# Routing's parts between the experts' products set further apart, VectorE's lower parts of the inner rows behind routing's answers, and GpSimd's fetches moved to match

## The chip, the cores and the metric

The kernel runs on one core of one Trainium2 chip. The metric is the device time of one execution in microseconds (us), the median of the runs shown. TensorE, VectorE, ScalarE and GpSimd each work through a queue of their own in order and wait for each other at semaphores; a wait holds everything behind it on its engine.

## The reference

Attention with a local window and eight global keys, then a dense layer pair with SiLU, then a layer of 8 experts to which 3072 tokens are assigned greedily. The last part, cut to what matters:

```python
logits = x @ w_gate                      # 3072 tokens, 8 experts, cap = 3072 / 8 = 384
order = np.argsort(-logits.flatten())
for idx in order:                        # best pairs first
    tok, e = idx // E, idx % E
    if assigned[tok] >= 0 or counts[e] >= cap:
        continue
    assigned[tok] = e
    counts[e] += 1
for e in range(E):                       # D = 512, F = 1024
    mask = assigned == e
    out[mask] = np.maximum(x[mask] @ w1[e], 0.0) @ w2[e]
```

## The kernel before

The first block (attention and the dense layers) ends at about 709 us and is not touched. The second block, `routed_experts`, computes the experts in the order in which they fill up, so that an expert can be computed while the next are still being routed.

**Products.** An expert is 56 products on TensorE, numbered m = 0 to 55 (`MM`). The first 32 are up products: inner row f = 0 to 7 (128 of the 1024 inner values) by four pieces of D. The last 24 are down products: token tile t = 0 to 2 by f = 0 to 7. A product is three matmuls, since float32 values are split in a high part (rounded) and a lower part (what is left): high by high, high by low, low by high. Product n of the whole run is p * 56 + m for expert p.

**Inner rows.** When inner row f is complete (product 4f+3), ScalarE writes `hidden_high` (L1585) and VectorE `hidden_low` (L1815, in `rest_hidden`). They share three PSUM banks (`UP_BANKS`), so inner row f+3 waits for `hidden_low` of f, and down product 32+f reads it.

**Routing.** Round r finds the next expert that fills, in 22 parts k: seven levels, each a count (even k, TensorE L1416; answered on VectorE by `find_reached`) and a digit (odd k, TensorE L1425; answered by `move_key` and `compare`, which writes `cmp` for the next count), then wins (`WINS`, answered by `fill`, which gives the weights' index), the sum of marks (`SUMS`, `list_them`), three parts on VectorE alone (`MARK` and two halves of `one_hot`), the list (`LIST`, 24 matmuls L1450, answered by `keep_list`, which gives the tokens' index), and `NEXT` and `KEY`, which prepare the next round on VectorE. Levels 0 to 3 have wide compares (31 values), 4 to 6 narrow ones (15 or 17). Round 0 is done before expert 0; rounds 1 to 7 stand between the products of experts 0 to 5, by a table of gaps: `gaps_of(r)` gives for each part how many products after the part before it stands. `parts_behind` maps a product's number to its parts. TensorE does them behind that product in `between`, and VectorE's queue has their answers in the same places, in `decide`.

**Tokens.** From expert 2 on the tokens of an expert are turned (transposed, L1484) in two halves between the down products of the one before, behind m = 39 and 47 (47 and 51 in expert 1); expert 1's are turned at its own start. ScalarE rounds them (L1566), VectorE writes `ex_low` (L1810, in `rest_tokens`), and product 0 waits for that.

**Fetches.** GpSimd writes the lower parts of the weights (`w_low`, L1358 for w1 and L1373 for w2) and issues the indirect DMAs for the next expert between them: w1 (L1334), the tokens (L1350, three issues) and w2 (L1340). `fetch_early(p, f)` sets in front of which of w2's eight rows f the first two stand; each waits for routing's index.

## Time and profile before

| | |
|---|---|
| median of 3 runs | 1079.76 us (1079.34 to 1079.78) |
| profiled execution, its time | 1080.13 us |
| its span, first to last instruction | 1078.4 us |
| granted TensorE clock, mean over the span | 0.987 |
| the experts' products | 751.0 us to the end |

The span lies inside the profiled execution's own time, 1.7 us shorter. PE is TensorE's matmuls and PEld its weight loads, DVE is VectorE, ACT ScalarE, POOL GpSimd. In a timeline row the bracket behind an instruction gives the idle time of the engine before it and what released it. Matmuls overlap, so the distance from start to start is the pace, not the duration.

### The profile page before, as it was taken

The page shows a single profiled execution, that of the slowest core. Times are in us where ns is not written, and L with a number is a line of the kernel's source. Part 1 is how long each engine was busy: PE and PEld are TensorE (multiplying, and loading weights), DVE is VectorE, ACT ScalarE, POOL GpSimd, SP SyncE. Part 2 cuts the span into 40 slices and gives each one's busy share as a digit, 9 for nine tenths or more (in the row PEclk, how much of TensorE's full clock was granted, in tenths as well). Part 3 has the DMA queues.
Part 4 walks back from the last instruction along what each step waited for, and adds up shares of the span by engine and source line. Part 5 has one row for each costly group of instructions (what it writes and reads, how often), then busy time and mean ns, then how long its engine had stood idle before and what let it go on. Part 6 is the DMA issues. An engine that isn't in the chain of part 4 may idle for free. (4 is left out here: it accounts for less than half of the span.)

```text
span 1078.4 us, 19852 instructions
## 1 busy us (share of the span) xinstructions
PE 1035.2 (96%) x7291; PEld 888.8 (82%) x7291; DVE 615.9 (57%) x2248; ACT 460.4 (43%) x1172; POOL 422.3 (39%) x466
## 2 busy tenths in 40 slices
PE   9899999999999999999999999957899999999998
PEld 7688888888888888888888889846677877779987
DVE  6754736474646556564747462546767768774110
ACT  4775444444444444444444443212233334234442
POOL 1363222222222222222222224214476577667773
PEclk9999999999999999999999999977999999999999
DMA  6653212121112120112112000005055245324420
GB/s 185 224 209 119 75 53 70 56 75 45 62 55 75 53 70 30 59 56 76 56 62 69 11 31 2 19 21 186 1 215 182 95 153 184 140 98 171 161 108 29
DMA packets 23248, 98.15 MB, mean 91 GB/s; under 512 B 3008, under 2 KB 5056, under 8 KB 20960
## 3 DMA queue, kind: packets, MB, share of 16 engines
q0 software_dynamic: 9824, 58.99, 15.3%
q1 hardware_dynamic: 13328, 37.90, 10.5%
q8 instruction: 58, 0.95, 0.4%
q14 instruction: 38, 0.31, 0.1%
HBM read 84.30 MB, written 12.85 MB: 90 GB/s over the span
## 5 line engine op out<-in xcount | busy, mean ns | idle before, releaser
L427 POOL TENSOR_TENSOR g_low<-g,g_high 128x256 fp32r<-128x256 f32 x192 | 155.3, 809 | 471.4 <-ACT g_high L646 471.3
L536 PE MATMUL up_ps<-x_high,w_high 128*128 128x256 f32 x768 | 227.6, 296 | 0.0
L536 PE MATMUL up_ps<-x_low,w_high 128*128 128x256 f32 x768 | 216.2, 281 | 0.0
L536 PE MATMUL up_ps<-x_high,w_low 128*128 128x256 f32 x768 | 215.1, 280 | 0.0
L814 DVE SCALAR_TENSOR_TENSOR g<-g,up_ps 128x256 f32<-128x256 f32 x192 | 80.4, 419 | 235.6 <-ACT g L639 235.6
L646 ACT ACTIVATE g_high<-g 128x256 fp32r<-128x256 f32 x192 | 80.3, 418 | 209.4 <-PE down_ps L549 140.3
L536 PEld LDWEIGHTS up_ps<-x_high,w_high 128*128 128x128 f32 x768 | 144.5, 188 | 10.7 <-issue 7.7
L549 PE MATMUL down_ps<-w_high,g_high 128*128 128x512 f32 x384 | 152.1, 396 | 0.0
L549 PE MATMUL down_ps<-w_high,g_low 128*128 128x512 f32 x384 | 151.4, 394 | 0.0
L549 PE MATMUL down_ps<-w_low,g_high 128*128 128x512 f32 x384 | 151.2, 394 | 0.0
L536 PEld LDWEIGHTS up_ps<-x_low,w_high 128*128 128x128 f32 x768 | 144.7, 188 | 2.8
L536 PEld LDWEIGHTS up_ps<-x_high,w_low 128*128 128x128 f32 x768 | 144.9, 189 | 0.0
L802 DVE CUSTOM_DVE_ANT_0 product<-x,w_raw 128x512 bf16<-128x512 f32 x176 | 132.8, 754 | 3.0
L639 ACT ACTIVATE g<-up_ps 128x256 f32<-128x256 f32 x192 | 73.4, 382 | 101.2 <-PE up_ps L536 99.3
L1373 POOL TENSOR_TENSOR w_low<-w_raw,w_high 128x512 fp32r<-128x512 f32 x64 | 82.1, 1288 | 58.3 <-ACT w_high L1561 58.1
L604 ACT ACTIVATE probs<-probs,neg_max 128x232 f32<-128x232 f32 (+1 forms) x184 | 85.1, 463 | 43.7 <-DVE neg_max L734 43.7
L1504 PE MATMUL eup_ps<-ex_high,w_high 128*128 128x384 f32 x256 | 91.3, 357 | 1.4 <-DVE ex_low L1810 1.4
L549 PEld LDWEIGHTS down_ps<-w_high,g_low 128*128 128x128 f32 x384 | 71.9, 187 | 17.7
L1504 PE MATMUL eup_ps<-ex_high,w_low 128*128 128x384 f32 x256 | 86.0, 336 | 0.0
L1504 PE MATMUL eup_ps<-ex_low,w_high 128*128 128x384 f32 x256 | 86.0, 336 | 0.0
L1358 POOL TENSOR_TENSOR w_low<-w_raw,w_high 128x512 fp32r<-128x512 f32 x64 | 80.1, 1287 | 3.6 <-ACT w_high L1554 3.4
L1521 PE MATMUL edown_ps<-w_high,hidden_high 128*128 128x512 f32 x192 | 79.5, 414 | 0.0
(217 smaller groups left out, 1826.5 us busy)
## 6 DMA issues: line engine op xcount, KB each, us to landing
qk_t<-qk_rows SPq DMA_DIRECT2D x20, 720.0 KB, 4.2
v_w<-v_win SPq DMA_DIRECT2D x40, 232.0 KB
w_raw<-weights SPq DMA_DIRECT2D x16, 512.0 KB, 5.4
x_rest<-x_any POOLq DMA_DIRECT2D x24, 256.0 KB, 3.0
x_rows<-x POOLq DMA_DIRECT2D x12, 512.0 KB, 3.2
w_raw<-gate_rows SPq DMA_DIRECT2D x1, 2048.0 KB, 6.8
qk_t<-qk_rows SPq DMA_DIRECT2D x3, 512.0 KB, 4.2
v_w<-v_win SPq DMA_DIRECT2D x8, 128.0 KB
```

The source lines that it names most:

```text
L427: pool.tensor_tensor(g_low[:, u % 2, :], g[:, u % 2, :], g_high[:, u % 2, :].bitcast(F32), ALU.subtract)\
L536: last = nc.tensor.matmul(up_ps[:, u % 2, 0:GT * P], a[:, f, w], x[:, grp % 2, c, :], start=k == 0, stop=k == 3 * C - 1)
L549: last = nc.tensor.matmul(down_ps[:, t, :], a[:, m % 2, t * P:(t + 1) * P], x[:, f, C * P:], start=f == 0 and k == 0, stop=f == FC - 1 and ...
L604: nc.scalar.activation(probs_of(u)[:, a, 0:width], probs_of(u)[:, a, 0:width], ACT.Exp, bias=neg_max[:, u % 3, a:a + 1], scale=-1.0, accum ...
L639: nc.scalar.activation(g[:, u % 2, :], up_ps[:, u % 2, 0:GT * P], ACT.Tanh, scale=0.5)\
L646: nc.scalar.activation(g_high[:, u % 2, :], g[:, u % 2, :], ACT.Copy).then_inc(g_high_ready, 1)
L802: v.tensor_tensor_reduce(out=product[:, :], in0=x2[:, t, :], in1=gate_all[:, e, :], scale=1.0, scalar=0.0, op0=ALU.mult, op1=ALU.add, accu ...
L814: v.scalar_tensor_tensor(g[:, u % 2, :], g[:, u % 2, :], 1.0, up_ps[:, u % 2, 0:GT * P], ALU.add, ALU.mult).then_inc(g_ready, 1)
L1358: pool.tensor_tensor(w1_low[:, f, :], w1_raw[:, p % 2, f, :], w1_high[:, f, :].bitcast(F32), ALU.subtract).then_inc(w1_low_ready, 1)
L1373: pool.tensor_tensor(w2_low[:, f, :], w2_raw[:, f, :], w2_high[:, f, :].bitcast(F32), ALU.subtract).then_inc(w2_low_ready, 1)
L1504: last = nc.tensor.matmul(up_ps[:, f % UP_BANKS, 0:CAP], w[:, f, c * P:(c + 1) * P], x[:, c, :], start=k == 0, stop=k == 3 * C - 1)
L1521: last = nc.tensor.matmul(down_ps[:, t, :], h[:, f, at], w[:, f, :], start=f == 0 and k == 0, stop=f == FC - 1 and k == 2)
```

## The change

The table of gaps is set anew: round 1's last levels have gaps of 2 where they had 1; from round 2 on the first count stands 5 products behind `KEY` instead of 4, from round 4 on 6; from round 4 on also the sixth count stands one product later and the list 3 products behind the last mark instead of 2. All parts behind a changed gap move with it: round 2's by 4 products, round 3's by 5, round 4's by 7 to 9, round 5's by 11 to 13, round 6's by 15 to 17, round 7's by 17 and 18. VectorE's `rest_hidden` now comes behind the answers at its product and one product later (4f+4 instead of 4f+3). GpSimd's early fetches stand in front of later rows of w2.

```diff
--- before.py
+++ after.py
@@ -1286,10 +1286,11 @@
 
 
         def gaps_of(r):
-            ends = [2, 3] + [3, 1, 1] + [2, 1, 2]
+            ends = [2, 3] + [3, 1, 1] + [3 if r >= 4 else 2, 1, 2]
             if r == 1:
-                return [2, 2] + [3, 1] * (UPPER - 2) + [2, 1, 3, 1] + [2, 1] * (NL - UPPER - 1) + ends
-            return [4, 2] + [3, 2] * (UPPER - 2) + [2, 2, 3, 2] + [2, 2] * (NL - UPPER - 1) + ends
+                return [2, 2] + [3, 1] * (UPPER - 2) + [2, 2, 3, 2] + [2, 2] * (NL - UPPER - 1) + ends
+            late = int(r >= 4)
+            return ([5 + late, 2] + [3, 2] * (UPPER - 2) + [2, 2, 3 + late, 2] + [2, 2] * (NL - UPPER - 1) + ends)
 
         parts_behind = {}
         behind = -1
@@ -1361,9 +1362,9 @@
             def fetch_early(p, f):
 
 
-                if p + 1 < E and f == {0: FC, 1: 5, 2: 4, 3: 2}.get(p, 1):
+                if p + 1 < E and f == {0: FC, 1: 6, 2: 5, 3: 4}.get(p, 3):
                     fetch_w1(p + 1)
-                if p + 1 < E and f == {0: FC, 1: FC, 2: 6, 3: 5}.get(p, 3):
+                if p + 1 < E and f == {0: FC, 1: FC, 2: 7, 3: 6, 6: 3}.get(p, 5):
                     fetch_tokens(p + 1)
 
             def rest_w2(p):
@@ -1825,10 +1826,11 @@
                     rest_tokens(p, 0)
                     rest_tokens(p, 1)
                 for m in range(MM):
-                    if m < FC * C and m % C == C - 1:
-                        rest_hidden(p, m // C)
                     for r, k in parts_behind.get(p * MM + m, ()):
                         decide(r, k)
+
+                    if 0 < m <= FC * C and m % C == 0:
+                        rest_hidden(p, m // C - 1)
                     if turned_behind(p, m) is not None:
                         rest_tokens(p + 1, turned_behind(p, m))
```

On VectorE, in the first products of expert 0: `short` and `enough` answer a count of round 1, `digit`, `notes_ps` and `cmp` a digit, `hidden_low` is the lower part of an inner row. Before:

```order
1387 L1664 TENSOR_TENSOR short<-places,route_ps 31x8
1388 L1664 TENSOR_TENSOR short<-short,route_ps 31x8 x2
1389 L1671 TENSOR_TENSOR enough<-route_ps,short 31x8
1390 L1815 SCALAR_TENSOR_TENSOR hidden_low<-eup_ps,hidden_high 128x384
1391 L1676 TENSOR_REDUCE digit<-route_ps 128x1
1392 L1684 TENSOR_SCALAR notes_ps<-notes_ps,digit 128x24
1393 L1650 TENSOR_TENSOR cmp<-notes_ps,qk_t 128x16x31
1394 L1650 TENSOR_TENSOR cmp<-notes_ps,qk_t 128x8x31
1395 L1664 TENSOR_TENSOR short<-places,route_ps 31x8
1396 L1664 TENSOR_TENSOR short<-short,route_ps 31x8 x2
1397 L1671 TENSOR_TENSOR enough<-route_ps,short 31x8
```

And in the changed kernel:

```order
1387 L1665 TENSOR_TENSOR short<-places,route_ps 31x8
1388 L1665 TENSOR_TENSOR short<-short,route_ps 31x8 x2
1389 L1672 TENSOR_TENSOR enough<-route_ps,short 31x8
1390 L1677 TENSOR_REDUCE digit<-route_ps 128x1
1391 L1685 TENSOR_SCALAR notes_ps<-notes_ps,digit 128x24
1392 L1651 TENSOR_TENSOR cmp<-notes_ps,qk_t 128x16x31
1393 L1651 TENSOR_TENSOR cmp<-notes_ps,qk_t 128x8x31
1394 L1816 SCALAR_TENSOR_TENSOR hidden_low<-eup_ps,hidden_high 128x384
1395 L1665 TENSOR_TENSOR short<-places,route_ps 31x8
1396 L1665 TENSOR_TENSOR short<-short,route_ps 31x8 x2
1397 L1672 TENSOR_TENSOR enough<-route_ps,short 31x8
```

The lower part of inner row 0 stood ahead of the answer to the digit; now it stands behind that answer and its two compares, ahead of the answer to the next count.

On TensorE, at the end of expert 0 and the start of expert 1: `route_ps` rows are routing's parts, the 9 and 3 matmuls with `ident` turn expert 1's tokens. Before:

```order
3897 L1416 MATMUL route_ps<-wants,cmp 128x32 x6
3898 L1521 MATMUL edown_ps<-w_high,hidden_high 128x512
3899 L1521 MATMUL edown_ps<-w_low,hidden_high 128x512
3900 L1521 MATMUL edown_ps<-w_high,hidden_low 128x512
3901 L1484 MATMUL eup_ps<-ident,x_g 128x128 x9
3902 L1484 MATMUL edown_ps<-ident,x_g 128x128 x3
3903 L1504 MATMUL eup_ps<-ex_high,w_high 128x384
3904 L1504 MATMUL eup_ps<-ex_low,w_high 128x384
```

And in the changed kernel:

```order
3896 L1522 MATMUL edown_ps<-w_high,hidden_high 128x512
3897 L1522 MATMUL edown_ps<-w_low,hidden_high 128x512
3898 L1522 MATMUL edown_ps<-w_high,hidden_low 128x512
3899 L1426 MATMUL route_ps<-enough,qk_t 128x8
3900 L1485 MATMUL eup_ps<-ident,x_g 128x128 x9
3901 L1485 MATMUL edown_ps<-ident,x_g 128x128 x3
3902 L1505 MATMUL eup_ps<-ex_high,w_high 128x384
3903 L1505 MATMUL eup_ps<-ex_low,w_high 128x384
```

A count of round 2 stood ahead of expert 0's last product; now a digit of that round stands behind it, directly ahead of the turn, and the count that it leads to comes three products into expert 1 (VectorE answers in the same order).

On GpSimd, in expert 2: `w_low` with L1373 (now L1374) are w2's lower parts, L1334 (L1335) fetches expert 3's w1, L1350 (L1351) its tokens, L1340 (L1341) its w2, L1358 (L1359) are w1's lower parts. Before:

```order
167 L1373 TENSOR_TENSOR w_low<-w_raw,w_high 128x512 x4
168 L1334 DMA w_raw<-w_rows,weight_index 128x4096
169 L1373 TENSOR_TENSOR w_low<-w_raw,w_high 128x512 x2
170 L1350 DMA x_g<-x_rows,token_index 128x512 x3
171 L1373 TENSOR_TENSOR w_low<-w_raw,w_high 128x512 x2
172 L1340 DMA w_raw<-w_rows,weight_index 128x4096
173 L1358 TENSOR_TENSOR w_low<-w_raw,w_high 128x512 x8
```

And in the changed kernel:

```order
167 L1374 TENSOR_TENSOR w_low<-w_raw,w_high 128x512 x5
168 L1335 DMA w_raw<-w_rows,weight_index 128x4096
169 L1374 TENSOR_TENSOR w_low<-w_raw,w_high 128x512 x2
170 L1351 DMA x_g<-x_rows,token_index 128x512 x3
171 L1374 TENSOR_TENSOR w_low<-w_raw,w_high 128x512
172 L1341 DMA w_raw<-w_rows,weight_index 128x4096
173 L1359 TENSOR_TENSOR w_low<-w_raw,w_high 128x512 x8
```

The fetch of w1 and that of the tokens each stand behind one more lower part of w2. In experts 3, 4 and 5 the fetch of w1 moves by two, and the tokens' by one or two.

## Rows read from the trace of the kernel before

**Rows 1.** The page, busy time: engine, busy us (share of the span), instructions.
```profile
PE 1035.2 (96%) x7291; PEld 888.8 (82%) x7291; DVE 615.9 (57%) x2248; ACT 460.4 (43%) x1172; POOL 422.3 (39%) x466
```

**Rows 2.** The page, the chain that ended last: share of the span by engine.
```profile
PE 24%; DVE 6%; ACT 1%; issue 1%; DMA 1%; POOL 0%; DVEq 0%
```

**Rows 3.** Stretches by expert: A:B us, length, busy PE, PEld, DVE, ACT, POOL, PEclk, DMA.
```profile
751.00:797.80 46.80, 42.51 (x280) 33.67 (x280) 33.59 (x137) 15.68 (x33) 27.50 (x24) 1.00 0.33 130
797.80:841.80 44.00, 40.96 (x267) 33.28 (x268) 32.93 (x130) 15.47 (x32) 33.30 (x29) 1.00 0.39 138
...
1006.70:1041.10 34.40, 34.40 (x182) 31.41 (x181) 6.51 (x12) 15.59 (x31) 28.04 (x24) 1.00 0.45 168
```

**Rows 4.** TensorE's waits, all experts: total us, times, longest.
```profile
PE route_ps L1416 <- DVE cmp L1650: 6.0, 10, 1.0
...
PEld route_ps L1425 <- DVE enough L1671: 6.8, 19, 0.7
```

**Rows 5.** TensorE timeline, first products and the last: start us, us, what.
```profile
750.99 0.41 PE L1504 MATMUL eup_ps<-ex_high,w_high 128*128 128x384 f32 x1 [0.95 <-DVE ex_low L1810]
...
751.94 0.34 PE L1504 MATMUL eup_ps<-ex_high,w_low 128*128 128x384 f32 x1
752.12 0.32 PE L1416 MATMUL route_ps<-wants,cmp 128*128 128x32 bf16 x6
752.28 0.42 PE L1504 MATMUL eup_ps<-ex_high,w_high 128*128 128x384 f32 x1
...
1073.43 0.39 PE L1521 MATMUL edown_ps<-w_high,hidden_high 128*128 128x512 f32 x1
```

**Rows 6.** TensorE timeline, expert 0: two counts and a digit of round 1.
```profile
755.92 0.45 PE L1416 MATMUL route_ps<-wants,cmp 128*128 128x32 bf16 x6 [0.62 <-DVE cmp L1650]
...
757.20 0.18 PE L1425 MATMUL route_ps<-enough,qk_t 128*128 128x8 bf16 x1 [0.20 <-DVE enough L1671]
...
759.33 0.45 PE L1416 MATMUL route_ps<-wants,cmp 128*128 128x32 bf16 x6 [0.25 <-DVE cmp L1650]
```

**Rows 7.** VectorE timeline between those two counts.
```profile
756.41 0.17 DVE L1664 TENSOR_TENSOR short<-places,route_ps 31x8 f32<-31x8 f32 x1 [0.31 <-PE route_ps L1416]
...
756.99 0.15 DVE L1671 TENSOR_TENSOR enough<-route_ps,short 31x8 bf16<-31x8 f32 x1
757.55 0.56 DVE L1815 SCALAR_TENSOR_TENSOR hidden_low<-eup_ps,hidden_high 128x384 fp32r<-128x384 f32 x1 [0.41 <-ACT hidden_high L1585]
758.03 0.16 DVE L1676 TENSOR_REDUCE digit<-route_ps 128x1 f32<-128x8 f32 x1
...
758.51 1.00 DVE L1650 TENSOR_TENSOR cmp<-notes_ps,qk_t 128x496 bf16<-128x496 f32 x2
```

**Rows 8.** TensorE timeline: two lists, a last count, a first count.
```profile
781.66 0.77 PE L1450 MATMUL route_ps<-ids,one_hot 128*32 128x24 bf16 x24
...
820.22 0.83 PE L1450 MATMUL route_ps<-ids,one_hot 128*32 128x24 bf16 x24 [0.97 <-DVE one_hot L1758]
...
848.93 0.33 PE L1416 MATMUL route_ps<-wants,cmp 128*128 128x32 bf16 x6 [0.91 <-DVE cmp L1650]
...
901.18 0.54 PE L1416 MATMUL route_ps<-wants,cmp 128*128 128x32 bf16 x6 [1.01 <-DVE cmp L1650]
```

**Rows 9.** TensorE timeline: expert 1's first product.
```profile
797.78 0.41 PE L1504 MATMUL eup_ps<-ex_high,w_high 128*128 128x384 f32 x1 [0.44 <-DVE ex_low L1810]
```

**Rows 10.** GpSimd timeline, expert 2: expert 3's w1 fetch, third token fetch.
```profile
856.51 0.99 POOL L1334 DMA_INDIRECT w_raw<-w_rows,weight_index  x1
...
863.72 0.95 POOL L1350 DMA_INDIRECT x_g<-x_rows,token_index  x1 [0.30 <-issue]
```

**Rows 11.** DMA view of 860 to 870: busy tenths, 0.25 us a digit.
```profile
DMA  7993999979499964959884984750000000000395
```

**Rows 12.** TensorE timeline, expert 2: the first turn of expert 3's tokens.
```profile
871.03 0.82 PE L1484 MATMUL eup_ps<-ident,x_g 128*128 128x128 f32 x6
```

**Rows 13.** The tile w_raw: issue of a weight fetch to its landing.
```profile
DMA to landing us min/median/max: 8.5/9.3/10.0
```

## The prediction

> **What bounds the kernel now.** I read the page first: TensorE is busy for 1035.2 us of the 1078.4 us span, 96% [rows 1], and it leads the chain that ended last; VectorE is the only other engine with a share worth naming in it, 6% against 1% or less each [rows 2]. So the time is TensorE's work plus what it waits for, and the waits are VectorE's. Then I cut the experts' part by expert. With routing between its products expert 0 takes 46.80 us and expert 1 44.00; expert 6, which has no routing part, takes 34.40 with TensorE never idle, at a granted clock of 1.00 in all three [rows 3]. From the first to the seventh expert that is 255.7 us (751.0 to 1006.7) where six times 34.40 would be 206.4: routing costs 49.3 us.
>
> How much of it is work? A count that finds its answer ready costs 0.16 us itself (752.12 to 752.28), and the next product's first matmul takes 0.42 instead of 0.34 [rows 5]: 0.25 us. A digit part, one small matmul with the same tail, I put at 0.14, the counting of wins at 0.45, the sum of marks at 0.15, the list (24 matmuls, 0.77 with its answer ready [rows 8]) at 0.89. A round is 7 counts, 7 digits and those three: 4.2 us. Rounds 1 to 6 are 25.5 and round 7, a sum and a list, 1.0; expert 1's turn at its own start costs 0.8 more than two turns between products. 49.3 - 27.3 = **22 us are waits**. The same comes out when the 448 products are laid start to start (first 750.99, last 1073.43 [rows 5]; up products at 0.525 us, three matmuls 0.175 apart, down products at 0.69) and what each part costs above its undisturbed price is summed: 21.8 us. The view of waits names their kinds, counts waiting for cmp and digits waiting for enough, 6.0 and 6.8 us as its largest rows with VectorE as releaser [rows 4]; it splits them between TensorE's two queues, so I size the terms start to start.
>
> **One digit closely.** In expert 0 a count begins at 755.92; VectorE starts on it at 756.41 and has its answer at 757.14, so the digit goes at 757.20 [rows 6, 7]: 1.28 us from count to digit, where a gap of one up product offers about 0.9. VectorE could take the digit's answer about 0.27 us later, at 757.47. But product 7 has just ended and a lower part of the inner rows stands ahead in its queue: it waits 0.41 for ScalarE, starts at 757.55, and the digit's answer is read at 758.03 [rows 7], 0.56 late. The next count goes at 759.33 [rows 6], 2.13 after the digit; three up products with the tail are 1.7, undelayed it needs 1.56. Both kinds of wait are here: the gap of 1 (0.44) and the lower part ahead (0.5).
>
> **Part by part, the order on VectorE.** Nothing is added or removed; the lower part moves behind an answer at the same product and one product on. If no answer falls at 4f+4 it still runs when ScalarE is done; only an answer at 4f+3 or 4f+4 gains. But an answer whose compare was just made is now followed by the lower part (0.5 us), so the following answer can be late: 0.1 behind a wide compare three products on, 0.25 behind a narrow one two on. Its readers are far: product 4(f+3) needs the bank, 7 products (3.7 us) after the new place, and the down products need f at 32+f. Where list and key stand ahead of it (rounds 4 and 5) VectorE comes to f=7 some 4.2 us after product 31, and product 39 wants it 5.0 after: covered, with 0.8 to spare.
>
> **The terms**, waits now and then, start to start:
> - Round 1's digits in expert 0: now 6.8 (cnt1 0.9, five digits at 0.45 to 0.6, three counts at 0.5 to 0.65, the last digit 1.3). Then the lower part is behind the answer; the three early digits keep a gap of 1 (0.54 each), levels 4 on have 2 (0.1 each), the last 0.5. Together 2.6. **Gain 4.2.**
> - Digits and wins of rounds 2 to 6: now 7.2, of which round 3's last count 1.1 and wins 0.8 (the count's idle is 0.91 in the row, the rest in weight loads [rows 8]). Then wins follow a last digit at 4f+4 or with no lower part ahead (0), last digits keep 0.1 to 0.5, narrow levels 0.1 to 0.15, a digit behind a turn in round 6 0.3: together 3.1. **Gain 4.1.**
> - Lists: now 3.2 (round 2 1.1, idle 0.97 in the row [rows 8]). From marks to list VectorE needs 3.2 us plus 0.5 for each lower part in between; 7 up products with the tail are 3.8. Rounds 4 on get 8, round 2's list now ends among down products, and no part of the four has more than one lower part inside. Only round 3 keeps 0.2. **Gain 3.0.**
> - First counts: now 4.5 (round 5's 1.4, idle 1.01 in its row [rows 8]). VectorE needs 4.6 us from the list's end, 5.1 to 5.7 with lower parts; seven up products are 3.7. Now 8 or 9 products, many of them down: 5.2 to 5.7. Round 6, all up, keeps 0.35. **Gain 4.15.**
> - Expert 1's first product now waits 0.44 for x_low [rows 9]. At its boundary VectorE now has a digit's answer and compare (1.5 us) ahead of the tokens' lower parts, where it had a count's (0.74). **Loss 0.5.**
> - The parts' own cost does not change with their place (0.25 either side).
>
> **GpSimd's fetches.** The answers come 4 to 17 products later, so the fetches must; a fetch in front of an answer would hold w_low behind it. The tightest is expert 2. Its w1 fetch goes at 856.51 and the turn that needs expert 3's tokens begins at 871.03 [rows 10, 12]: 14.5 us. One row of w2 later is 2.1, the waits that go are 1.5, the parts no longer between 0.4: 10.5 us are left. A weight fetch lands in 8.5 to 10.0 us [rows 13], and the tokens, behind it in the same queue, were in at 866.8 (27 busy digits [rows 11]), 3.0 after their third issue at 863.72 [rows 10] and 1.8 after w1 by the 8.5. So 10.3 to 11.8 are needed: a margin of 0.2 or a stall of 1.3. I take **0.3 lost**, near the low end, since w1 and tokens were both in 10.3 us after the w1 fetch (866.8 - 856.5). Experts 3 to 5 start from 19 us and keep 13; w1's own use, by ScalarE before that turn, has 5 us.
>
> The Trainium skill (DMA: Bandwidth & Descriptors, the section Anatomy of one DMA) fits a transfer as 2.0 us plus its bytes over 436e3 per us. By it a 2 MB fetch takes 6.8 us and the tokens 2.6, the estimate for the margin is over 2 us, and the sum would be 0.3 us lower. The rows are slower than that fit, and the rows stand in the sum.
>
> **Sum.** 4.2 + 4.1 + 3.0 + 4.15 - 0.5 - 0.3 = 14.65 us. The profiled execution took 1080.13 us for its span of 1078.4, so the span should be 1063.8; the median shown is 1079.76, 0.4 less than the profiled time: 1079.76 - 14.65 = **1065.1 us**. Waits left: 21.8 down to about 7.
>
> **Rivals.**
> - *Waits move instead of going.* The lower part now stands between a compare and the next answer at each narrow level, and VectorE, busy 33 of 44 us in an expert [rows 3], never catches up. For it: 0.5 us against slacks of 0.1 to 0.2. Against: expert gaps of 2 down products have 0.3 spare. If half the digit gain and a third of the rest come back (4.1 + 2.4), the gain is 8: 1071.6.
> - *All waits go.* If the lags I charge for the postponed lower part (about 3 us) are absorbed, the gain is 18 to 20: 1061.
> - *Tokens or weights land late.* The stall of 1.3 at expert 2 and one like it at expert 1 (its token list is now at product 34 of 56, the turn at 47): gain 12, 1067.8, inside the main range.
> - *Slower: GpSimd is held.* A fetch that stands before routing's answer blocks w_low of w2, and TensorE needs those from product 32. The answer for w1 is due 0.5 to 1.5 us before GpSimd comes to the fetch, and behind it lie 5 us until product 32+f. It decides only where routing is over 6 us late; then each of five experts stalls, and over 3 us each (15 in all) are needed to be slower: 1083 with 3.6 each. Nothing in the traces is that late.
> - *No change.* If the experts' pace were set by weights (GpSimd) and not by VectorE. Expert 6 runs the same weights in 34.40 with TensorE full [rows 3], against it.
>
> **Chances.** Main case 0.64 (its own range 1062 to 1069), half moved 0.20 (1069 to 1075), all waits go 0.09 (1058 to 1062), held or stalled beyond before 0.04, no change 0.03. The range 1061.5 to 1071.5 leaves out about 0.2. Under 0.2% (2 us) a measurement of this kernel cannot be told from no change: faster 0.93, same 0.03, slower 0.04.
>
> **What would show it.** Expert 0 near 42.6 us (46.8 - 4.2 + 0.5 - the half microsecond of parts and marks that moves on), expert 1 near 40.5, expert 6 still 34.40. VectorE rows of expert 0: digit directly after enough, hidden_low behind cmp. No list with over 0.3 us idle before it, first counts under 0.4. A DMA releaser on the turns of expert 2 would show the fetch term wrong, w_low as a releaser in down products the held case, and digits still waiting 0.5 in rounds 2 to 6 the half-moved one. I am wrong above all if the lags behind the postponed lower part add up from one answer to the next.

## The result and the profile after

The changed kernel takes **1064.85 us** (median of 4 runs, 1064.1 to 1065.54) where the kernel before takes 1079.77 on the same chip (4 runs, 1079.34 to 1080.2): a ratio of 0.9861, interval 0.9849 to 0.9872. Forecast were 1065.1 us and a range of 1061.5 to 1071.5. The profiled run took 1065.54 us with a span of 1063.7.

The page after, the same two lines as [rows 1, 2]:

```profile
PE 1031.3 (97%) x7291; PEld 888.7 (84%) x7291; DVE 614.3 (58%) x2248; ACT 461.2 (43%) x1172; POOL 422.2 (40%) x466
...
PE 27%; DVE 4%; POOL 1%; issue 1%; ACT 0%; DVEq 0%; POOLq 0%
```

The same instructions are there, 7291 on TensorE and 2248 on VectorE, and VectorE's part in the chain fell from 6% to 4%. The stretches of experts 0, 1 and 6, as in [rows 3]:

```profile
751.00:793.60 42.60, 40.73 (x274) 33.37 (x274) 32.40 (x133) 16.12 (x33) 28.22 (x24) 1.00 0.38 142
793.60:833.90 40.30, 39.80 (x266) 33.15 (x267) 31.32 (x126) 15.08 (x30) 31.41 (x28) 1.00 0.40 144
...
992.00:1026.40 34.40, 34.40 (x182) 31.40 (x181) 6.51 (x12) 15.67 (x31) 27.95 (x24) 1.00 0.42 161
```

Expert 0 went from 46.80 to 42.60 us, expert 1 from 44.00 to 40.30, and expert 6, without routing, stayed at 34.40: the forecast's marks were 42.6, near 40.5 and 34.40. From the first product to the last matmul the experts' part is 308.17 us (751.02 to 1059.19) where it was 322.89: 14.7 us shorter, all that the span lost. What lies ahead of the experts did not move.

One digit closely, the same place as [rows 6, 7]. TensorE's two parts, then VectorE's rows:

```profile
755.17 0.32 PE L1417 MATMUL route_ps<-wants,cmp 128*128 128x32 bf16 x6
...
756.46 0.18 PE L1426 MATMUL route_ps<-enough,qk_t 128*128 128x8 bf16 x1 [0.36 <-DVE enough L1672]
```

```profile
756.25 0.15 DVE L1672 TENSOR_TENSOR enough<-route_ps,short 31x8 bf16<-31x8 f32 x1
756.68 0.17 DVE L1677 TENSOR_REDUCE digit<-route_ps 128x1 f32<-128x8 f32 x1 [0.28 <-PE route_ps L1426]
...
757.17 1.00 DVE L1651 TENSOR_TENSOR cmp<-notes_ps,qk_t 128x496 bf16<-128x496 f32 x2
758.08 0.55 DVE L1816 SCALAR_TENSOR_TENSOR hidden_low<-eup_ps,hidden_high 128x384 fp32r<-128x384 f32 x1
```

The digit's answer is now read 0.22 us after the digit's start (0.83 before: 757.20 to 758.03), the lower part stands behind cmp, and it waits for nothing there: ScalarE's part was done at 756.63. The digit itself still waits, 0.36 in its row, since its gap is one up product. TensorE's other three places, to be laid beside [rows 9, 8, 12]: expert 1's first product, round 3's list, the first turn of expert 3's tokens; and its last matmul.

```profile
793.59 0.41 PE L1505 MATMUL eup_ps<-ex_high,w_high 128*128 128x384 f32 x1 [0.78 <-DVE ex_low L1811]
...
852.28 0.45 PE L1451 MATMUL route_ps<-ids,one_hot 128*32 128x24 bf16 x12 [0.30 <-DVE one_hot L1759]
...
860.83 0.88 PE L1485 MATMUL eup_ps<-ident,x_g 128*128 128x128 f32 x6 [0.16 <-DMA x_g<-x_rows,token_index]
...
1059.19 0.39 PE L1522 MATMUL edown_ps<-w_high,hidden_low 128*128 128x512 f32 x1
```

The waits of TensorE's matmuls in the experts' part (total, times, longest), where [rows 4] had 6.0 for cmp alone:

```profile
PE route_ps L1426 <- DVE enough L1672: 1.0, 3, 0.4
PE route_ps L1426 <- DVE enough L1670: 1.0, 2, 0.5
...
PE eup_ps L1505 <- DVE ex_low L1811: 0.8, 1, 0.8
PE route_ps L1451 <- DVE one_hot L1759: 0.3, 1, 0.3
PE eup_ps L1485 <- DMA x_g<-x_rows,token_index: 0.2, 1, 0.2
```

Of the counts' waits for cmp one is left, 0.2 us in the weight loads. A view of waits splits a wait between TensorE's two queues, so all sums below are worked out as in the prediction: the time from one product's first matmul to the next one's, less 0.525 or 0.69 for the product, less each part's undisturbed price, with one set of prices for every kernel. The split between the groups depends on the prices by some tenths of a microsecond: with the cheapest row of each kind as its price rounds 2 to 6 come to 8.4 before and 4.0 after. The last row, the length of the experts' part, does not depend on them.

| waits by group, and the experts' part as a whole, us | before | after | order alone | gaps alone |
|---|---|---|---|---|
| round 1's counts and digits | 6.6 | 2.4 | 4.6 | 5.7 |
| rounds 2 to 6, digits and wins | 8.6 | 4.8 | 3.8 | 12.2 |
| lists | 3.3 | 0.4 | 2.1 | 1.7 |
| first counts | 4.5 | 0.3 | 3.9 | 0.9 |
| experts' part, whole length | 322.9 | 308.2 | 314.3 | 320.8 |

### The profile page after: what moved, and what is told of

It reads as the page before. It is cut to its first block and busy times, and to the rows that moved or that the text cites. A ratio compares the mean times of both kernels' runs of the same rounds, so it can differ in the third digit from the quotient of the medians.

```text
span 1063.7 us, 19849 instructions
## 1 busy us (share of the span) xinstructions
PE 1031.3 (97%) x7291; PEld 888.7 (84%) x7291; DVE 614.3 (58%) x2248; ACT 461.2 (43%) x1172; POOL 422.2 (40%) x466
## 5 line engine op out<-in xcount | busy, mean ns | idle before, releaser
L1374 POOL TENSOR_TENSOR w_low<-w_raw,w_high 128x512 fp32r<-128x512 f32 x64 | 82.0, 1291 | 47.2 <-ACT w_high L1562 44.9
L1359 POOL TENSOR_TENSOR w_low<-w_raw,w_high 128x512 fp32r<-128x512 f32 x64 | 80.1, 1286 | 0.7 <-issue 0.5
L549 PEld LDWEIGHTS down_ps<-w_high,g_high 128*128 128x128 f32 x384 | 72.2, 188 | 8.6 <-POOL g_low L427 0.4
```

Source lines behind the costliest of these rows:

```text
L549: last = nc.tensor.matmul(down_ps[:, t, :], a[:, m % 2, t * P:(t + 1) * P], x[:, f, C * P:], start=f == 0 and k == 0, stop=f == FC - 1 and ...
L1359: pool.tensor_tensor(w1_low[:, f, :], w1_raw[:, p % 2, f, :], w1_high[:, f, :].bitcast(F32), ALU.subtract).then_inc(w1_low_ready, 1)
L1374: pool.tensor_tensor(w2_low[:, f, :], w2_raw[:, f, :], w2_high[:, f, :].bitcast(F32), ALU.subtract).then_inc(w2_low_ready, 1)
```

## The experiments

Twelve kernels, grouped by question. "Start to start" names the sums just described.

**Order alone.** The kernel before with only the third hunk of the change (the lower part behind the answers, one product later). Against the changed kernel:

```diff
-            ends = [2, 3] + [3, 1, 1] + [3 if r >= 4 else 2, 1, 2]
+            ends = [2, 3] + [3, 1, 1] + [2, 1, 2]
...
-            return ([5 + late, 2] + ...
+            return [4, 2] + ...
...
(and the fetches at before's rows)
```

> The kernel before with one edit: VectorE's lower part of an inner row comes behind the answers and one product later; gaps and fetches as before. My theory (the lower part ahead of an answer was itself a cause of waits, worth about a third of the gain): 4 to 6.5 us faster than the kernel before, ratio 0.994 to 0.996, and in the trace the counts of round 1 lose their 0.5 us waits while lists and first counts keep theirs. Rival (the gaps do it all; the lower part behind a compare delays the next answer by as much as it saved): 0 to 2 us, ratio 0.998 to 1.000.

Measured: 1070.72 us (1070.29 to 1071.28), ratio 0.9919 [0.9904, 0.9935], experts' part 314.3, so 8.6 us of the 14.7. More than expected. Round 1's digits gave 2.0, the digits and wins of the later rounds 4.8, the lists 1.2. The first counts hardly moved (4.5 to 3.9): they need products, not an order. With the new gaps the later rounds' digits wait 1.0 more than here (4.8 for 3.8); the gaps earn their place at the lists, the first counts and round 1.

**Gaps and fetches alone.** The changed kernel with the lower part ahead of the answers again:

```diff
+                    if m < FC * C and m % C == C - 1:
+                        rest_hidden(p, m // C)
                     for r, k in parts_behind.get(p * MM + m, ()):
                         decide(r, k)
-                    if 0 < m <= FC * C and m % C == 0:
-                        rest_hidden(p, m // C - 1)
```

> The changed kernel with one edit undone: the lower part stands ahead of the answers again, at product 4f+3; gaps and fetches as in the changed kernel. My theory: the lists and first counts keep their gain of about 7 us, round 1's digits and the last digits and wins get waits of 0.5 back; 8 to 11 us faster than before, ratio 0.990 to 0.993, 4 to 6 us behind the changed kernel. Rival (gaps do it all): 13 to 15 us faster than before, ratio 0.986 to 0.988.

Measured: 1077.36 us (1076.82 to 1079.09), ratio 0.9984 [0.9975, 0.9993], experts' part 320.8: 2.1 us, a clear miss. The lists and first counts do gain 5.3 us, as expected, and round 1 another 0.9. But rounds 2 to 6 wait 12.2 us where they waited 8.6. The later places have put other parts behind a product 4f+3 or 4f+4, and each new wait over 0.4 is at such a place. One of them, TensorE and then VectorE:

```profile
765.88 0.18 PE L1426 MATMUL route_ps<-enough,qk_t 128*128 128x8 bf16 x1
768.56 0.32 PE L1417 MATMUL route_ps<-wants,cmp 128*128 128x32 bf16 x6 [0.82 <-DVE cmp L1651]
```

```profile
765.49 0.15 DVE L1672 TENSOR_TENSOR enough<-route_ps,short 15x8 bf16<-15x8 f32 x1
766.60 0.56 DVE L1816 SCALAR_TENSOR_TENSOR hidden_low<-eup_ps,hidden_high 128x384 fp32r<-128x384 f32 x1 [0.95 <-ACT hidden_high L1586]
767.07 0.15 DVE L1677 TENSOR_REDUCE digit<-route_ps 128x1 f32<-128x8 f32 x1
...
768.00 0.60 DVE L1651 TENSOR_TENSOR cmp<-notes_ps,qk_t 128x240 bf16<-128x240 f32 x2
```

VectorE stands idle for 0.95 us on ScalarE with the digit's answer lying in PSUM behind it: the digit went at 765.88, is read at 767.07, and the next count waits 0.82. A gap set to fit VectorE's work is of no use while something that waits stands ahead in its queue. So the two edits don't add: 8.6 and 2.1 alone, 14.7 together.

**Before's fetches.** The changed kernel, with GpSimd's fetches of w1 and the tokens back at their old rows:

```diff
-                if p + 1 < E and f == {0: FC, 1: 6, 2: 5, 3: 4}.get(p, 3):
+                if p + 1 < E and f == {0: FC, 1: 5, 2: 4, 3: 2}.get(p, 1):
                     fetch_w1(p + 1)
-                if p + 1 < E and f == {0: FC, 1: FC, 2: 7, 3: 6, 6: 3}.get(p, 5):
+                if p + 1 < E and f == {0: FC, 1: FC, 2: 6, 3: 5}.get(p, 3):
                     fetch_tokens(p + 1)
```

> The changed kernel with GpSimd's fetches in front of the same rows of w2 as before, so that they wait for routing's later answers and hold w2's lower parts behind them. This is the case I called held. My prediction's slack (it decides only beyond 6 us) would make it free: within 1 us of the changed kernel. A closer count says that in experts 3 and 4 the tokens' fetch is answered at product 27 or so, the five lower parts behind it are then done 10 us later, and TensorE waits 1 to 2 us in each for w_low in the first down products: 2 to 4 us slower than the changed kernel, ratio to before 0.988 to 0.990, and the 0.4 us wait for tokens at expert 2 is gone.

Measured: 1066.93 us (1066.47 to 1067.51), ratio 0.9881 [0.9866, 0.9896], experts' part 310.7, 2.5 us longer than the changed kernel's. The waits of its matmuls have a row that neither kernel before nor after has:

```profile
PE edown_ps L1522 <- POOL w_low L1374: 1.6, 6, 0.4
```

Down products 37 and 38 of experts 2, 3 and 4 wait 0.44 to 0.55 each start to start; that is 2.8 us more than in the changed kernel, and the turn in expert 2 gives 0.24 back, since it no longer waits for its tokens. A fetch in front of its answer blocks GpSimd's queue, and the weights' lower parts behind it come late: the held rival's mechanism, at a small price.

**The last level's enough straight from PSUM.** This began with a row of the changed kernel that I had not expected. VectorE at the end of round 2, and GpSimd over the same time:

```profile
807.54 0.15 DVE L1669 TENSOR_TENSOR margins<-route_ps,short 17x8 f32<-17x8 f32 x1
807.73 0.80 DVE L1670 TENSOR_SCALAR enough<-margins 17x8 bf16<-17x8 f32 x1
```

```profile
807.22 1.28 POOL L1374 TENSOR_TENSOR w_low<-w_raw,w_high 128x512 fp32r<-128x512 f32 x1 [1.20 <-ACT w_high L1562]
```

An operation over 17 x 8 elements takes 0.80 us where its neighbour takes 0.15, and ends at 808.53, within 0.03 of the end of GpSimd's w_low (808.50). Over the kernels before and after and the first three experiments there are 35 of these: 24 take 0.16, and the 11 long ones (0.49 to 0.80) all begin inside a w_low and end with it. (In two of the 11, one in the kernel before and one in order alone, the next w_low follows at once and the operation gets through all the same.) So the operation reads PSUM instead:

```diff
-                    link(v.tensor_tensor(margins[0:reach, :], counts_at[0:reach, 0:E], missing, ALU.subtract))
-                    v.tensor_scalar(enough[0:reach, :], margins[0:reach, :], 0.0, None, ALU.is_ge).then_inc(enough_known, 1)
+                    v.tensor_tensor(margins[0:reach, :], counts_at[0:reach, 0:E], missing, ALU.subtract)
+                    v.tensor_tensor(enough[0:reach, :], counts_at[0:reach, 0:E], missing, ALU.is_ge).then_inc(enough_known, 1)
```

> The changed kernel with the last level's answer taken straight from the counts (a tensor-tensor compare that reads PSUM) instead of from margins in SBUF (a tensor-scalar from SBUF to SBUF), which in the traces takes 0.16 us, but 0.5 to 0.8 wherever it starts while GpSimd runs a w_low, ending within 0.1 us of it. Theory (the operation is held by GpSimd's running instruction, as both want the same port): the new operation takes 0.15 in all six rounds, the digits of rounds 2 and 6 lose their 0.65 us waits, 1.3 to 2 us faster than the changed kernel, ratio to before 0.984 to 0.985. Rival (the long ones have another cause, such as a late count, and come back on the new operation): 0.3 us or less.

Measured: 1062.62 us (1062.32 to 1063.31), ratio 0.9845 [0.9832, 0.9859], experts' part 306.4, 1.8 us shorter. Round 6's last level, VectorE and then GpSimd:

```profile
954.90 0.15 DVE L1669 TENSOR_TENSOR margins<-route_ps,short 17x8 f32<-17x8 f32 x1
954.99 0.14 DVE L1670 TENSOR_TENSOR enough<-route_ps,short 17x8 bf16<-17x8 f32 x1
```

```profile
954.59 1.29 POOL L1374 TENSOR_TENSOR w_low<-w_raw,w_high 128x512 fp32r<-128x512 f32 x1 [1.73 <-ACT w_high L1562]
```

It begins inside a w_low again and takes 0.14. The last digits of rounds 2 and 6 waited 0.66 and 0.67 and now 0.01, those of rounds 3 and 4 0.22 and now 0.09. Not all of the 1.8 us is the hold: the edit also lets the comparison start without waiting for margins, so that from the start of margins to the end of enough it takes 0.23 us where even an operation that nothing held took 0.35. The two rounds with a held operation gained 0.65 and 0.66, and rounds 1, 3 and 4 gained 0.12 or 0.13 each: 1.3 us for the hold and its share of the shorter chain, about 0.4 for the rest.

**Behind, but not later.** The lower part behind the answers, at its old product 4f+3:

```diff
-                    if 0 < m <= FC * C and m % C == 0:
-                        rest_hidden(p, m // C - 1)
+                    if m < FC * C and m % C == C - 1:
+                        rest_hidden(p, m // C)
```

> The changed kernel with the lower part behind the answers but not one product later: at product 4f+3, after that product's answers. Theory (an in-order queue: while the lower part waits 0.4 to 0.8 us for ScalarE it holds the answer that falls on the next product, 4f+4): the answers at 4f+3 keep their gain, those at 4f+4 wait again, of which the changed kernel's places have some 12 (round 1's two last digits, last digits of rounds 3 and 4, last counts and wins of rounds 2 and 6): 2 to 5 us slower than the changed kernel, ratio to before 0.988 to 0.991, waits at parts whose predecessor stands at 4f+4. Rival (standing behind is all that matters): within 0.7 us of the changed kernel.

Measured: 1067.02 us (1066.97 to 1067.15), ratio 0.9887 [0.9871, 0.9902], experts' part 310.6, 2.4 us longer. The waits are back where an answer stands at 4f+4 (last counts of rounds 1, 3 and 4 0.54 to 0.58 each, three wins 0.3 each): there the lower part, one product ahead, still waits for ScalarE in front of it. From the lower part ahead (320.8) to behind (310.6) to behind and later (308.2): the first step is 10.2 us, the second 2.4.

**w1's fetch one row earlier in expert 2.**

```diff
-                if p + 1 < E and f == {0: FC, 1: 6, 2: 5, 3: 4}.get(p, 3):
+                if p + 1 < E and f == {0: FC, 1: 6, 2: 4, 3: 4}.get(p, 3):
```

> The changed kernel with expert 3's w1 fetch in front of w2's row 4 instead of row 5 in expert 2. Theory (the 0.36 us wait at the first turn in expert 2 is for tokens that queue behind that w1 transfer): the wait goes, 0.3 to 0.5 us faster in expert 2. Rival (the tokens' own issue is the late one, at 858.1 for the third with 3 us to land): the wait stays at 0.3 to 0.4, since the tokens' fetch waits for routing's list and not for w1. The whole difference is below what the times can tell; the turn's row decides.

Measured: 1064.64 us (1064.19 to 1065.04), ratio 0.9865 [0.985, 0.988]: no change. GpSimd's first token fetch, and TensorE's turn:

```profile
853.19 0.97 POOL L1351 DMA_INDIRECT x_g<-x_rows,token_index  x1 [0.78 <-DVE token_index L1772]
...
855.73 0.95 POOL L1351 DMA_INDIRECT x_g<-x_rows,token_index  x1 [0.30 <-issue]
```

```profile
859.67 0.88 PE L1485 MATMUL eup_ps<-ident,x_g 128*128 128x128 f32 x6 [0.38 <-DMA x_g<-x_rows,token_index]
```

Counted from the experts' first product (749.68 here, 751.02 in the changed kernel) w1 went 1.4 us earlier (846.84 for 849.63), but the third token fetch at the same point (855.73 for 857.13), since the first of them waits 0.78 for its list, and the turn still waits. In the nine kernels whose turn waits for the tokens it begins 3.7 to 4.2 us after the third token fetch is issued, whenever w1 went.

**Round 1's early gaps.** Two up products for each digit as in the later rounds, given back behind round 1 so that the later rounds keep their places:

```diff
             if r == 1:
-                return [2, 2] + [3, 1] * (UPPER - 2) + [2, 2, 3, 2] + [2, 2] * (NL - UPPER - 1) + ends
+                return ([2, 2] + [3, 2] * (UPPER - 2) + [2, 2, 3, 2] + [2, 2] * (NL - UPPER - 1) +
+                        [2, 2] + [3, 1, 1] + [1, 1, 2])
             late = int(r >= 4)
-            return ([5 + late, 2] + ...
+            return ([5 + late - int(r == 2), 2] + ...
```

> The changed kernel with gaps of 2 instead of 1 in front of round 1's second, third and fourth digit, and the three products taken back where round 1 has slack (sum of marks, list, first count of round 2), so that rounds 2 to 7 stand where they stood. Theory (a count's answer takes 1.28 us, a gap of 1 offers 0.9): the three waits of 0.6 us go, and no new one above 0.2 comes: 1.5 to 2 us faster than the changed kernel, ratio to before 0.984 to 0.985. Rival (the wait is only put off, to the list or round 2's first count, which now have less room): 0.5 us or less.

Measured: 1063.43 us (1062.48 to 1063.93), ratio 0.9854 [0.9839, 0.987], experts' part 306.65, 1.5 us shorter. Digits 1 to 3 waited 0.59, 0.64 and 0.59 and wait 0.01 each: one up product is too short for an answer of 1.3 us, two are enough.

**Together.** The last two with the direct enough, w1 earlier, and round 3's list one product later:

```diff
-            ends = [2, 3] + [3, 1, 1] + [3 if r >= 4 else 2, 1, 2]
+            ends = [2, 3] + [3, 1, 1] + [3 if r >= 3 else 2, 1, 2]
...
-            return ([5 + late - int(r == 2), 2] + ...
+            return ([5 + late - int(r in (2, 4)), 2] + ...
```

> All that helped so far in one kernel: the last level's answer straight from the counts, round 1's gaps, expert 3's w1 one row earlier, and round 3's list one product further with one product taken from round 4's first count. If the terms add (1.8 + 1.7 + 0.4 + 0.4): 4.0 to 4.5 us faster than the changed kernel, 1060.5 or ratio 0.982 to before. If they collide in VectorE's queue: half of it.

Measured: 1062.23 us (1060.99 to 1064.56), ratio 0.9843 [0.9829, 0.9856], experts' part 305.3: 2.9 us shorter than the changed kernel's, not the 4 and more of the expectation. Every wait on VectorE that was aimed at went. But the later list made GpSimd wait for its token list, and the turn paid (wait 0.9 start to start, and product 38 another 0.44 for w_low):

```profile
851.84 0.97 POOL L1352 DMA_INDIRECT x_g<-x_rows,token_index  x1 [0.89 <-DVE token_index L1773]
```

**List, then tokens.** The same with w1 back in its row and one product taken from round 3's first gap instead of round 4's:

```diff
-            return ([5 + late - int(r in (2, 4)), 2] + ...
+            return ([5 + late - int(r in (2, 3)), 2] + ...
...
-                if p + 1 < E and f == {0: FC, 1: 6, 2: 4, 3: 4}.get(p, 3):
+                if p + 1 < E and f == {0: FC, 1: 6, 2: 5, 3: 4}.get(p, 3):
```

> The kernel of all terms together, with expert 3's w1 back in front of row 5 and the product for round 3's longer list gap taken from round 3's own first count instead of round 4's, so that its list stands at product 28 of expert 2 as in the changed kernel. Theory (the tokens of expert 3 are bound by routing's answer to that list: list, answer, three issues, 3 us to land; in the kernel with all together the list stood one product later and the turn waited 0.9, w_low 0.4): the turn waits 0.1 or nothing, no w_low wait; experts' part 3.8 to 4.2 us shorter than the changed kernel's 308.2, ratio to before 0.982 to 0.983. Rival (the terms collide in VectorE's queue anyway): 3 us shorter or less, with new waits over 0.3 at counts or digits.

Measured: 1061.23 us (1060.65 to 1061.35), ratio 0.9823 [0.981, 0.9836], experts' part 305.0, which is 3.2 us shorter than the changed kernel's where 3.8 to 4.2 were expected. GpSimd no longer waits for the list (the 0.42 us left before its first token fetch have no releaser), but the turn still waits 0.59 in its row. The third token fetch, and the turn:

```profile
853.39 0.95 POOL L1352 DMA_INDIRECT x_g<-x_rows,token_index  x1 [0.30 <-issue]
```

```profile
857.55 0.87 PE L1486 MATMUL eup_ps<-ident,x_g 128*128 128x128 f32 x6 [0.59 <-DMA x_g<-x_rows,token_index]
```

**Both fetches.** That kernel with w1 a row earlier again:

```diff
-                if p + 1 < E and f == {0: FC, 1: 6, 2: 5, 3: 4}.get(p, 3):
+                if p + 1 < E and f == {0: FC, 1: 6, 2: 4, 3: 4}.get(p, 3):
```

> The kernel before it (list, then tokens) with expert 3's w1 fetched in front of row 4 again. There the tokens no longer waited for routing's list, but landed 2.1 us after a w1 that took 9.1, and the turn waited 0.8. Theory (the turn waits for the later of two things, w1's landing plus 2 us and the third token issue plus 3.4, so that each fix alone was hidden by the other): now both are early, the turn's wait falls to 0.2 or less, experts' part 304.3 to 304.5 us, 0.5 shorter than in the kernel before it, ratio to before 0.981 to 0.983. Rival (the wait is the turn's own and not of the tokens' coming): it stays at 0.7 or more.

Measured: 1060.75 us (1060.22 to 1061.18), ratio 0.9826 [0.9813, 0.984], experts' part 304.5. The turn waits 0.35 start to start (0.79 in the kernel just before), above the 0.2 expected and the same as the changed kernel's 0.36; the third token fetch went at 853.64 and the turn at 857.33, so 3.69 after it instead of 4.16. By the trace that fetch landed at 857.28, just ahead of the turn; w1 had landed at 853.18, before it was issued, where in the kernel just before w1 landed at 855.40, 2.0 us after it. The half microsecond between the two lies inside the spread of their runs. It has the lowest median of all, 4.1 us below the changed kernel's median and 18.7 below that of before on its chip.

**What holds a small operation up.** The changed kernel with four operations behind each lower part of experts 6 and 7, 17 x 8 each, whose results nothing uses:

```diff
+                if p >= 6:
+                    link(v.tensor_scalar(enough[0:17, :], margins[0:17, :], 0.0, None, ALU.is_ge))
+                    link(v.tensor_scalar(full_rank[0:17, :], closed[0:17, :], 0.0, None, ALU.is_ge))
+                    link(v.tensor_tensor(won[0:17, :], margins[0:17, :], places[0:17, :], ALU.is_ge))
+                    link(v.tensor_tensor(short[0:17, :], margins[0:17, :], closed[0:17, :], ALU.is_ge))
```

(`closed` lies in PSUM, `margins` and `places` in SBUF.)

> The changed kernel with four small operations of 17 partitions by 8 elements behind each of the 16 lower parts of experts 6 and 7, where no routing runs and GpSimd makes a w_low of 1.29 us each about then; results unused. A: tensor-scalar from SBUF; B: the same from PSUM; C: tensor-tensor with both inputs in SBUF; D: tensor-tensor with one of them in PSUM. Theory (only an operation that takes the port that GpSimd uses is held): A takes 0.16, or if it starts inside a w_low up to 0.8, ending within 0.05 us of the w_low's end; B and D are never held; C is held or not by its own kind, which this shows. Rival (any small VectorE operation is slow beside GpSimd): B and D are stretched as well. Time: 0 to 1 us slower than the changed kernel.

Measured: 1072.55 us in one run, 7.7 above the changed kernel, not 0 to 1. VectorE, GpSimd, and TensorE behind them:

```profile
1004.46 6.29 DVE L1819 TENSOR_SCALAR enough<-margins 17x8 bf16<-17x8 f32 x1
1010.78 0.15 DVE L1820 TENSOR_SCALAR full_rank<-notes_ps 17x8 f32<-17x8 f32 x1
...
1011.88 5.05 DVE L1819 TENSOR_SCALAR enough<-margins 17x8 bf16<-17x8 f32 x1
```

```profile
1004.44 6.28 POOL L1374 TENSOR_TENSOR w_low<-w_raw,w_high 128x512 fp32r<-128x512 f32 x5
...
1011.97 4.93 POOL L1359 TENSOR_TENSOR w_low<-w_raw,w_high 128x512 fp32r<-128x512 f32 x4
```

```profile
1018.14 0.79 PE L1522 MATMUL edown_ps<-w_high,hidden_high 128*128 128x512 f32 x1 [5.16 <-DVE hidden_low L1816]
1018.73 0.63 PE L1522 MATMUL edown_ps<-w_low,hidden_high 128*128 128x512 f32 x1
```

A 17 x 8 comparison stood for 6.29 us: it ended not with the w_low that began with it, but when GpSimd first paused, five w_low later. The two operations with an input in PSUM took 0.15 us in all 32 rows; nine of these, all of the tensor_scalar, began inside a w_low. TensorE idled for 5.16 us and its matmuls then took 0.63 instead of 0.39; the stretches say why (their last three columns are the granted clock, the DMA engines' share and GB/s):

```profile
1012.00:1018.00 6.00, 0.96 (x3) 0.49 (x3) 5.86 (x5) 0.00 (x0) 4.90 (x4) 0.82 0.90 336
1018.00:1024.00 6.00, 5.86 (x19) 4.84 (x20) 1.72 (x7) 3.39 (x7) 1.32 (x2) 0.61 0.03 14
```

The granted clock fell to the lower level, 1.2 GHz, at 1015.9, while TensorE stood idle, and was back at 1.00 from 1022.7 on. Start to start the experts' part is 8.3 us longer than the changed kernel's: 5.4 for this wait, 0.5 for one before it, and 2.2 for matmuls at the lower level.

**The same with two SBUF inputs.** Only the third operation is left, so that it stands where the first one stood:

```diff
+                if p >= 6:
+                    link(v.tensor_tensor(won[0:17, :], margins[0:17, :], places[0:17, :], ALU.is_ge))
```

> The changed kernel with one small VectorE operation behind each lower part of the inner rows in experts 6 and 7 (16 in all): a comparison of two SBUF tiles, 17 x 8, whose result nothing uses. In the probe of four operations the single-input one, standing first, was held for 6.29 and 5.05 us where GpSimd had five and four w_low back to back, and the two-input one, standing third, for at most 1.03 us; but it never met such a chain. Here it stands first, where the other stood. Theory A (each operation is held until GpSimd next pauses, whatever its kind): two rows of 5 to 6.3 us again in expert 6's down products, TensorE waits some 5 us at one place, time 7 to 8 us above the changed kernel (1072 to 1073). Theory B (the comparison of two SBUF tiles waits only for the w_low that runs): no row over 1.35 us, TensorE waits under 0.5 us there, time within 1 us of the changed kernel's (1064 to 1066). I hold B likelier (0.6), since the two-input rows so far all ended within 0.02 us of a w_low's end; but at those places GpSimd paused right then, so they speak for neither.

Measured: 1069.45 us in one run, 4.6 above the changed kernel. VectorE, then GpSimd:

```profile
1004.74 6.33 DVE L1819 TENSOR_TENSOR won<-margins,places 17x8 f32<-17x8 f32 x1
...
1012.23 10.05 DVE L1819 TENSOR_TENSOR won<-margins,places 17x8 f32<-17x8 f32 x1
```

```profile
1004.75 6.30 POOL L1374 TENSOR_TENSOR w_low<-w_raw,w_high 128x512 fp32r<-128x512 f32 x5
1011.32 0.96 POOL L1341 DMA_INDIRECT w_raw<-w_rows,weight_index  x1 [0.27 <-POOL w_low L1374]
```

The theory that I held likelier fell: the comparison of two SBUF tiles was held for 6.33 us over five w_low and 10.05 over eight. The time is below the 1072 expected: the operation held for 6.33 us cost TensorE nothing here, and the one held for 10.05 made it wait once, for tokens' lower parts behind it. That wait, then two stretches:

```profile
PE eup_ps L1485 <- DVE ex_low L1811: 3.1, 1, 3.1
...
1018.00:1024.00 6.00, 2.92 (x16) 2.28 (x15) 5.77 (x4) 0.98 (x3) 5.27 (x5) 1.00 0.10 41
1024.00:1030.00 6.00, 6.00 (x21) 4.79 (x20) 0.56 (x1) 0.49 (x2) 0.99 (x1) 0.72 0.23 87
```

TensorE waited 3.1 us at once, until 1022.93. Its clock was still at 1.00 up to 1024.0 and then at the lower level until 1027.4, with its matmuls at 0.63 instead of 0.39. Of the 4.8 us by which the experts' part is longer than the changed kernel's, 3.3 are the wait and 1.6 the slower matmuls.

## Why the prediction was right

The sum forecast 14.65 us and the span lost 14.7, and the terms hold one by one in size, all start to start. (One slip of the working changes nothing: six rounds of parts are 25.3 us, not 25.5.)

- *Round 1's digits*, 4.2 forecast: 4.3. The three early digits keep 0.59 to 0.64 each where I had put 0.54.
- *Digits and wins of rounds 2 to 6*, 4.1 forecast: 3.8. By the one set of prices they start from 8.6 and keep 4.8, not 7.2 and 3.1. Of what stays, 1.3 us is the held enough in rounds 2 and 6, which the forecast did not know and which the change did not touch: in the kernel before it is held in rounds 1, 2 and 6.
- *Lists*, 3.0 forecast: 2.9, with 0.45 left at round 3 alone (the forecast named round 3, with 0.2).
- *First counts*, 4.15 forecast: 4.2, with 0.27 left at round 6 (0.35 forecast).
- *Expert 1's first product*, 0.5 lost: 0.3 (0.44 to 0.78 in its row).
- *Tokens at expert 2*, 0.3 lost: 0.36, with DMA as the releaser of the turn. That releaser was the forecast's own sign that the fetch term is wrong. The size was right and the reason at most half: I measured the margin from w1's fetch, and moving that alone changed nothing, with the tokens' fetch tied to the list that GpSimd waits for (0.74 us, of which 0.42 stand there even with the list ready). With the list early and w1 in its old row the turn waited 0.79, and with both early 0.35 again. That the size came out is luck.

Three things the forecast did not say. It named the lags behind the postponed lower part as the greatest danger; they came to little (0.15 behind the narrow levels). It added gains part by part, with lists and first counts put down to the gaps, and said nothing of what the gaps lose elsewhere while the lower part still stands ahead: the gaps alone give 2.1 us. I had expected 8 to 11 of them when I had the result in hand, so the right total had hidden a wrong split. And its held rival was mis-sized in one step: "it decides only where routing is over 6 us late". With the old fetches the waits on w_low are there at this change's own delays, and cost 2.5 us net. The sign never hung on it, but the second hunk of the change has its place by that row.

The rivals: no half of the digit gain came back, not all waits went (7.9 of 23.0 stay by these sums, 0.7 more at turns and boundary), and none of w_low's rows waits in down products.

What stays open: why the turn comes 3.7 us after the tokens' third issue in four kernels and 3.9 to 4.2 in five. How long before it w1 went does not order them (7.5 and 9.1 us in the four, 7.1 to 9.0 in the five). In the run list, then tokens w1 landed after the third issue and in both fetches before it, but w1 one row earlier and together sent w1 almost as far ahead as both fetches did (8.9 and 9.0 us for 9.1) and their turns came 3.9 and 4.0 us after the issue. No kernel measured the two transfers apart.

## What to carry to other kernels

In an engine's queue the instruction that waits for another engine belongs behind those whose input is ready, and only then are gaps worth tuning: each edit was measured alone here, and the gaps alone were worth a seventh of what both were. When a wait goes, look at what the freed engine now asks for sooner, since here the fetches had to move with routing's answers (2.5 us), and the tokens became what a turn waits for. And a right sum is no proof of its terms: undo each part of a change by itself.

## What the hardware showed

**A small VectorE operation can be held over several GpSimd instructions.** Held were a tensor_scalar of 17 x 8 from SBUF to SBUF (0.49 to 0.80 us in the routing, 0.96 to 6.29 in the first probe) and a comparison of two SBUF tiles (0.96 to 1.03 against single w_low, 6.33 and 10.05 against five and eight). An operation with an input in PSUM never was: the comparison that reads its counts from PSUM (`enough<-route_ps,short`) took 0.14 to 0.16 in all of the more than 200 rows of these kernels that begin inside a w_low. Nor was a tensor_scalar over one element a partition from SBUF to SBUF (`sides`, `weight_index`: 0.20 to 0.22 in over 100 such rows). In a fetch's issue a single-input one was held once (0.35 instead of 0.15, ending at 1000.65 where the fetch's row ends at 1000.67) and ran through another in 0.15; the two-input one ran through four in 0.14 or 0.15 and took 0.21 once. The Trainium skill (SBUF — State Buffer, the section Who interferes with whom) has a port pair that VectorE and GpSimd share under an exclusive lock, which these two kinds of operation can take and one with at most one SBUF input outside the two-port modes does not. The trace agrees on which operations are held. That section of the Trainium skill has the loser wait for the winner's instruction; in four rows of the probes it waited for four, five, five and eight instructions, and the measurement decides.

What ends a hold is open. Those four began within 0.1 us of the start of their chain's first w_low and ended where the chain did. But in the kernel before one that began in the middle of a w_low got free with its end, though the next followed without a pause, and order alone has another such row. VectorE, then GpSimd:

```profile
961.36 0.71 DVE L1669 TENSOR_SCALAR enough<-margins 17x8 bf16<-17x8 f32 x1
```

```profile
960.73 2.56 POOL L1358 TENSOR_TENSOR w_low<-w_raw,w_high 128x512 fp32r<-128x512 f32 x2
```

The operation ended at 962.07, the pair of w_low at 963.29. Written from PSUM, with the shorter chain that this brings, the last enough gains 1.8 us in this kernel.

**The clock after an idle stretch.** In the first probe TensorE ran no matmul for some 5 us (5.16 in its row), and the granted clock was at the lower level from 1015.9, still inside that stretch, to 1022.7. In the second it waited 3.1, and the clock was at the lower level from 1024.0, when matmuls had been running again for 1.1 us, to 1027.4. The slower matmuls cost 2.2 and 1.6 us on top of the waits.
